# Soft mixture-of-experts stage on one Trainium2 core: token tiles stored tile by tile, transposed through a ring of four quarter-buffers, and two expert-weight loads issued at other places

## Chip, cores, metric

One core of a Trainium2 chip. The metric is the device time in microseconds (us) of one execution of the whole program. Below, TensorE (PE) does matmuls and transposes, VectorE is DVE, ScalarE is ACT, GpSimd is POOL, and SP is the engine whose only work here is to issue DMAs.

## What is computed

Three stages in a row, all in float32: attention over 32 heads with pooled queries, a soft mixture of experts (MoE), and a gated feed-forward layer. The change lies where the second begins.

```python
def _attn_ref(q, k, v):                  # B,H,S,D = 4,8,1152,64; queries pooled by 2 -> 576 rows a head
    q_pool = q.reshape(B, H, S // 2, 2, D).mean(axis=3)
    attn = softmax(q_pool @ k.T / sqrt(D))
    return attn @ v
...
def _moe_ref(x, phi, w1, w2):            # x 2304x512 tokens, 8 experts of 4 slots, w1 8x512x1024, w2 8x1024x512
    logits = x @ phi
    d = np.exp(logits - logits.max(0)); d /= d.sum(0)
    slot_input = d.T @ x                 # 32 slots
    h = np.maximum(slot_input[e] @ w1[e], 0.0); slot_out[e] = h @ w2[e]      # for each expert e
    c = np.exp(logits - logits.max(1)); c /= c.sum(1)
    return c @ slot_out
...
def _moe2_ref(x, w_gate, w_val, w_out, rms_g):                                # d_ff = 1536
    xn = x / rms(x) * rms_g
    return (silu(xn @ w_gate) * (xn @ w_val)) @ w_out
```

## The kernel before

**Attention** runs over 16 pairs of heads (`attention`, an unrolled start, a loop, an unrolled end). Its result stays in SBUF as `x_nat`: 2304 tokens are five tiles (`NI` = 5: four of 128 tokens and a tail of 64) of each of the four batches, 512 channels each. Before the change a pair's five tiles lie side by side in `x_nat`, so one tile's channels are spread over the whole buffer.

**The MoE stage** (`rest`, `slots_tensor`, `slots_scalar`, `slots_vector`, `slots_sync`) first needs logits, so PE transposes each token tile (L1050, `token_transposes`) into one of six PSUM banks, ACT and DVE in turn copy the banks to the SBUF buffers `xt` (L1129, L1130), and PE multiplies them by `phi` (L1063, `logits`), four batches at a time in four column strips of the array. Before the change a job is one batch of one tile with its four channel blocks `c`, and the logits of a whole tile (16 matmuls) follow the 16 transposes of the tile after it. When the last logits are there (`lt_step`), DVE takes the maxima, ACT the exponentials, PE sums the tokens by their weights, tile by tile (L1096, `z_ps`), and `slots_done` says that the 32 slot inputs are ready. Then come the experts, four at a time (`g` = 0, 1): first layer (L1442), transposes, second layer (L1481); and then shares of `w_gate` and `w_val` (L1497), and the main loop of the feed-forward stage (L1624).

**Weights.** All expert weights, 33.5 MB, come from HBM by DMAs issued in program order from SP's one queue. Those of the first four experts go to seven slots and `w2_last` while attention ends. Those of the other four have to wait for a free place; their first layers are loaded by channel block `c`, four experts together, 2 MB each: `w1_first` (c = 0) in attention's block, then `w1_third` (c = 2, in pieces), `w1_second` (c = 1, on top of `x_nat`), then `slots_of_four` (c = 3 and the second layers), `weights`, and the feed-forward weights `w_gv` and `wo_raw`. Each has its wait in SP's program, below.

**Between the two stages** stands a block end (L1908) at which all five engines wait for each other: an engine arrives when its instructions of the block are issued or done, SP when it has issued its last DMA.

```python
        sp.wait_ge(group_ready, s_groups.upto(NPAIR - 1, 1))
        sp.dma_start(mem.w1_first[:], mem.w1_v[4:8, :, 0, :].rearrange("e p f -> p e f")).then_inc(mem.w1_first_in, 16)
    ...
    def slots_sync(sp):
        sp.wait_ge(lt_step, NI)
        sp.dma_start(w1_next[2][:, 0:3, :], ...)
        sp.wait_ge(z_ready, 1)
        sp.dma_start(w1_next[1], ...)
        sp.wait_ge(slots_done, 1)
        sp.dma_start(w1_next[2][:, 3, :], ...)
```

Of the kernel before, what the change touches and what calls it, by code (L numbers as in the profile page):

```python
# [6 lines left out]
P = 128  # L7
# [160 lines left out]
def attention(nc, mem, q, k, v):  # L168
# [221 lines left out]
    def _(sp):  # L390
# [74 lines left out]
        sp.dma_start(mem.w1_first[:], mem.w1_v[4:8, :, 0, :].rearrange("e p f -> p e f")).then_inc(mem.w1_first_in, 16)  # L465

# [314 lines left out]
    def _(dve):  # L781
# [77 lines left out]
        def normalise(at, k):  # L859
# [4 lines left out]
            if at.step is None:  # L864
                where = bass.ds((at.pair - 1) * NI * P, NI * P)
            else:
                where = bass.ds(at.step * (2 * NI * P) + (at.pair - 1) * NI * P, NI * P)
            x_pair = x_nat[:, where].rearrange("p (i h d) -> p i h d", i=NI, h=2)
# [50 lines left out]
def rest(nc, mem, w_gate, w_val, w_out, out):  # L919
# [15 lines left out]
    w1_third = mem.sb("w1_third", [P, 4, F1], FP32)  # L935
    assert mem.at == end_r3
    mem.at = third
# [3 lines left out]
    w1_in = [mem.w1_first_in] + [sem(f"w1_in{c}") for c in range(1, KT)]  # L941
# [36 lines left out]
    mem.at = mem.x_end - 4 * NPAIR * NI * P  # L978
    hid = mem.sb("hid", [P, F1], FP32)
# [3 lines left out]
    w1_second = mem.sb("w1_second", [P, 4, F1], FP32)  # L983
    mem.at -= SLOT
    comb_cat = mem.sb("comb_cat", [P, NI * B, 4, NS], F32R)
    plain_t = mem.sb("plain_t", [P, NTOK + P - TAIL], F32R)
# [15 lines left out]
    x_tiles = x_nat[:, :].rearrange("p (b c i d) -> p b i c d", b=B, c=HP, i=NI)  # L1002
# [22 lines left out]
    xt_jobs = [[(b, i)] for i in range(NF) for b in range(B)] + [[(0, NF), (1, NF)], [(2, NF), (3, NF)]]  # L1025
# [4 lines left out]
    def jobs_of(i):  # L1030
        return range(B * i, B * i + B) if i < NF else range(B * NF, B * NF + 2)
# [9 lines left out]
    def slots_tensor(pe):  # L1041
        def token_transposes(i):
            for n in jobs_of(i):
                if n >= NTB:
                    pe.wait_ge(xt_out_v if n % 2 else xt_out_a, (n - NTB) // 2 + 1)
                rows = rows_of(i)
                for m, (b, _) in enumerate(xt_jobs[n]):
                    for c in range(KT):
                        at = rows * (KT * m + c)
                        last = nc.tensor.transpose(banks[:, n % NTB, at:at + rows], x_tiles[0:rows, b, i, c, :],  # L1050
                                                   ident[0:rows, 0:rows])
                last.then_inc(xt_ready, 1)

        def logits(i):
            if i == 0:
                pe.wait_ge(small_in, 32)
            done = (jobs_of(i)[-1] + 1) // 2
            pe.wait_ge(xt_out_a, done)
            pe.wait_ge(xt_out_v, done)
            rows = rows_of(i)  # L1060
            for c in range(KT):
                for b in range(B):
                    last = nc.tensor.matmul(lt_ps[32 * b:32 * b + 32, P * i:P * i + rows], phi_sb[:, c, :],  # L1063
                                            xt[i % 2][:, c, b, 0:rows],
                                            start=(c == 0), stop=(c == KT - 1), tile_position=(0, 32 * b))
            last.then_inc(lt_step, 1)

        token_transposes(0)
        for i in range(1, NI):
            token_transposes(i)  # L1070
            logits(i - 1)
# [49 lines left out]
    def xt_job_out(engine, copy, n):  # L1121
# [3 lines left out]
        if i >= 2:  # L1125
            engine.wait_ge(lt_step, i - 1)
# [838 lines left out]
```

## Time and profile before

| | |
|---|---|
| three runs, us | 803.42, 804.03, 807.40 (median 804.03) |
| the profiled execution | 807.56 us, of which its span is 805.6 us (1.96 us lie around it) |
| PE, DVE, ACT busy | 786.8, 500.0, 460.9 us |
| granted clock of PE, mean | 0.991 of full |

The span is the time from the first instruction of the program to the last. Attention fills it up to about 540 us, the MoE stage and the preparation of the feed-forward weights go to about 625 us, the feed-forward loop to the end. PE is busy nearly throughout, but "busy" counts a matmul from its start to its modelled end.

### The profile page before, as it was taken

How to read it: one execution, taken by the hardware profiler on the slowest of the kernel's cores; microseconds unless marked ns; L12 is line 12 of the kernel's file. 1: busy time of each engine (PE TensorE's matmuls, PEld its weight loads, DVE VectorE, ACT ScalarE, POOL GpSimd, SP SyncE). 2: the span in 40 equal slices, each digit the busy share in tenths (PEclk: the TensorE clock that was granted, in tenths of full speed). 3: DMA queues.
4: the chain of work that ended last, by engine and by line, in shares of the span. 5: the costliest groups of instructions: out<-in, count | busy, mean ns of one | idle time of the engine just before them, and what ended most of it. 6: DMA issues, size and time to landing. Idle time of an engine off the chain costs nothing. (4 is left out here: it accounts for less than half of the span.)

```text
span 805.6 us, 16312 instructions
## 1 busy us (share of the span) xinstructions
PE 786.8 (98%) x5286; PEld 585.6 (73%) x5286; DVE 500.0 (62%) x967; ACT 460.9 (57%) x873; POOL 181.3 (23%) x243
## 2 busy tenths in 40 slices
PE   7999999999999999999999999989998999999997
PEld 7777777777777777777777777766344888888876
DVE  6766667666666676666756666644325566666665
ACT  5676676676766667666767676642123454434333
POOL 6351331522414325133152240000002330000000
PEclk9999999999999999999999999999998899999999
DMA  8539747365383463744836518586997001010010
GB/s 229 124 88 289 202 104 180 81 150 119 90 201 82 123 157 78 175 103 102 188 74 148 122 34 239 219 290 227 401 400 303 0 1 53 1 52 21 33 52 27
DMA packets 83032, 112.02 MB, mean 139 GB/s; under 512 B 45361, under 2 KB 47409, under 8 KB 82481
## 3 DMA queue, kind: packets, MB, share of 16 engines
q1 hardware_dynamic: 82832, 111.24, 48.7%
q8 instruction: 24, 0.39, 0.2%
q10 hardware_dynamic: 160, 0.26, 0.1%
q14 instruction: 16, 0.12, 0.0%
HBM read 71.37 MB, written 4.72 MB: 94 GB/s over the span
## 5 line engine op out<-in xcount | busy, mean ns | idle before, releaser
L579 PE MATMUL scores<-k_stack,q_stack 128*128 128x384 f32 x960 | 275.1, 376 | 2.8 <-DVE q_stack L796 2.4
L766 ACT COPY pt<-tbank 128x384 f32<-128x384 f32 x288 | 138.2, 480 | 152.8 <-PE tbank L516 152.7
L516 PE MATMUL tbank<-ident,probs 128*128 128x128 f32 x1296 | 219.5, 278 | 0.4 <-ACT probs L738 0.3
L516 PEld LDWEIGHTS tbank<-ident,probs 128*128 128x128 f32 x1296 | 156.5, 140 | 67.8 <-issue 41.9
L738 ACT ACTIVATE probs<-scores,neg_max 128x1152 f32<-128x1152 f32 x144 | 175.9, 1222 | 7.4 <-DVE neg_max L836 3.0
L612 PE MATMUL obank<-pt,v_in 128*64 128x320 f32 (+1 forms) x1152 | 167.3, 417 | 0.9 <-ACT o_t L753 0.9
L832 DVE TENSOR_REDUCE row_max<-scores 128x1 f32<-128x384 f32 x144 | 80.1, 556 | 117.0 <-PE scores L579 115.5
L579 PEld LDWEIGHTS scores<-k_stack,q_stack 128*128 128x128 f32 x960 | 147.8, 191 | 3.8 <-ACT k_stack L378 2.6
L825 DVE TENSOR_REDUCE row_max<-scores 128x1 f32<-128x768 f32 x144 | 136.6, 948 | 2.2 <-PE scores L579 1.6
L612 PEld LDWEIGHTS obank<-pt,v_in 128*64 128x64 f32 x1152 | 72.0, 136 | 58.1 <-issue 25.8
L887 DVE COPY pt<-tbank 128x384 f32<-128x384 f32 x144 | 80.2, 557 | 36.8 <-PE tbank L516 34.1
L343 POOL TENSOR_TENSOR k_hi<-k_lo,one 128x512 fp32r<-128x512 f32 (+1 forms) x45 | 37.2, 826 | 279.6 <-ACT k_lo L683 262.2
L1721 ACT CAST h_hi<-hid 128x512 fp32r<-128x512 f32 (+1 forms) x60 | 34.7, 578 | 102.2 <-DVE hid L1858 102.2
L1624 PE MATMUL banks<-wo_hi,h_hi 128*128 128x512 f32 x216 | 86.2, 399 | 0.6 <-DVE h_lo L1864 0.4
L1624 PE MATMUL banks<-wo_lo,h_hi 128*128 128x512 f32 x216 | 85.1, 394 | 0.0
L1624 PE MATMUL banks<-wo_hi,h_lo 128*128 128x512 f32 x216 | 84.9, 393 | 0.0
L1864 DVE TENSOR_TENSOR h_lo<-hid,h_hi 128x512 fp32r<-128x512 f32 (+1 forms) x60 | 38.3, 639 | 37.9 <-ACT h_hi L1721 37.9
L1809 DVE TENSOR_TENSOR scaled<-banks,inv_rms 128x512 f32<-128x512 f32 (+1 forms) x60 | 38.2, 636 | 27.8 <-PE banks L1536 27.1
L1624 PEld LDWEIGHTS banks<-wo_hi,h_hi 128*128 128x128 f32 x216 | 41.1, 190 | 11.4 <-DVE h_lo L1864 3.3
L1624 PEld LDWEIGHTS banks<-wo_hi,h_lo 128*128 128x128 f32 x216 | 41.1, 190 | 8.8
L1624 PEld LDWEIGHTS banks<-wo_lo,h_hi 128*128 128x128 f32 x216 | 41.2, 191 | 8.1
L348 POOL TENSOR_TENSOR k_lo<-k_lo,k_hi 128x512 fp32r<-128x512 f32 (+1 forms) x45 | 45.4, 1008 | 3.5
(217 smaller groups left out, 702.7 us busy)
## 6 DMA issues: line engine op xcount, KB each, us to landing
weights<-in_moe_w SPq DMA_DIRECT2D x7, 2048.0 KB, 11.4
v_in<-in_v SPq DMA_DIRECT2D x16, 576.0 KB, 4.0
k_in<-in_k SPq DMA_DIRECT2D x30, 288.0 KB, 4.9
k_stack<-k_hi SPq DMA_DIRECT2D x30, 288.0 KB, 3.6
k_stack<-k_lo SPq DMA_DIRECT2D x30, 288.0 KB, 3.6
q_in<-in_q SPq DMA_DIRECT2D x14, 512.0 KB, 5.1
slots_of_four<-in_moe_w SPq DMA_DIRECT2D x12, 512.0 KB, 11.2
q_stack<-q_hi SPq DMA_DIRECT2D x30, 144.0 KB, 3.3
```

The costliest lines, as they stand in the source:

```text
L348: last = ops.tensor_tensor(low[:, cols], low[:, cols].bitcast(FP32), high[:, cols].bitcast(FP32), ALU.subtract)
L516: last = nc.tensor.transpose(tbank[:, bank, cols], src, ident[0:rows, 0:rows])
L579: last = nc.tensor.matmul(scores[:, bank, 0:CH], q_stack[at.par][:, h, order, cols], k_stack[at.par][:, h, keys], start=(x == 0), stop=(x ...
L612: last = nc.tensor.matmul(obank[rows, 0:GROUP_WIDTH[group]], v_in[:, par, h, D * kt:D * kt + D], pt[group][:, h, kt, :], start=(kt == 0), ...
L738: nc.scalar.activation(probs[:, odd, :].rearrange("p (c k) -> p c k", c=3), scores[:, first:first + 3, 0:CH], ACT.Exp, bias=neg_max[:, odd ...
L766: nc.scalar.copy(pt_out(at, e), pt_from(at, e)).then_inc(out_by_act, 1)
L825: nc.vector.tensor_reduce(row_max[:, odd, 0:1], scores[:, first:first + 2, 0:CH], axis=AX.XY, op=ALU.max).then_inc(partial_max, 1)
L832: nc.vector.tensor_reduce(row_max[:, odd, 1:2], scores[:, 2, 0:CH], axis=AX.X, op=ALU.max).then_inc(partial_max, 1)
L887: nc.vector.tensor_copy(pt_out(at, e), pt_from(at, e)).then_inc(out_by_dve, 1)
L1624: last = nc.tensor.matmul(y_ps[:, t, :], a[:, f % 3, cols], w[:, f, :], start=(f == 0 and x == 0), stop=(f == NFT - 1 and x == 2))
L1809: nc.vector.tensor_tensor(scaled[:, f % 2, 0:width], gv_ps[:, f % 2, 0, 0:width], inv_rms[:, columns(n)], ALU.mult).then_inc(scaled_done, 1)
L1864: nc.vector.tensor_tensor(h_lo[:, f % 3, 0:width], hid2[:, f % 2, 0:width], h_hi[:, f % 3, 0:width].bitcast(FP32), ALU.subtract).then_inc( ...
```

## The change

`x_nat` is stored tile by tile: `[P, NI, NPAIR * P]`, so that the first two tiles are one contiguous stretch, exactly as large as `w1_second`, and `w1_second` is put there. A new semaphore `z_step` is raised when the token sums of tiles 0 and 1 are done, and the load of `w1_second` waits for it and no longer for `z_ready`.

The transposed tokens go through a ring of four buffers, each with one channel block of four batches (2 KB a partition, half the room in all). A job is now one (tile, channel block), four transposes and four logit matmuls, and PE's order is four jobs of transposes, then one job's logits and one job's transposes in turn. There are 20 jobs; `lt_step` counts all of them. This frees the place of two of the four experts of `w1_third` during attention: their load, 1 MB, is issued in attention's block, right behind `w1_first`; the third expert's is issued after the last logits, alone.

```diff
         sp.dma_start(mem.w1_first[:], mem.w1_v[4:8, :, 0, :].rearrange("e p f -> p e f")).then_inc(mem.w1_first_in, 16)
+        sp.dma_start(mem.w1_third[:, 0:2, :], mem.w1_v[4:6, :, 2, :].rearrange("e p f -> p e f")).then_inc(mem.w1_third_in, 16)
...
-            x_pair = x_nat[:, where].rearrange("p (i h d) -> p i h d", i=NI, h=2)
+            x_pair = x_nat[:, :, where].rearrange("p i (h d) -> p i h d", h=2)
...
-    xt = [mem.sb(f"xt{n}", [P, KT, B, P], FP32) for n in range(2)]
+    xt = mem.sb("xt", [P, 4, B, P], FP32)
...
-    xt_jobs = [[(b, i)] for i in range(NF) for b in range(B)] + [[(0, NF), (1, NF)], [(2, NF), (3, NF)]]
+    xt_jobs = [(i, c) for i in range(NI) for c in range(KT)]
...
     def slots_sync(sp):
-        sp.wait_ge(lt_step, NI)
-        sp.dma_start(w1_next[2][:, 0:3, :], mem.w1_v[4:7, :, 2, :].rearrange("e p f -> p e f")).then_inc(w1_in[2], 16)
-        sp.wait_ge(z_ready, 1)
+        sp.wait_ge(lt_step, len(xt_jobs))
+        sp.dma_start(w1_next[2][:, 2, :], mem.w1_v[6, :, 2, :]).then_inc(w1_in[2], 16)
+        sp.wait_ge(z_step, 1)
         sp.dma_start(w1_next[1], mem.w1_v[4:8, :, 1, :].rearrange("e p f -> p e f")).then_inc(w1_in[1], 16)
         sp.wait_ge(slots_done, 1)
         sp.dma_start(w1_next[2][:, 3, :], mem.w1_v[7, :, 2, :]).then_inc(w1_in[2], 16)
...
+        def token_transposes(n):
+            i, c = xt_jobs[n]
+            rows = rows_of(i)
+            if n >= NTB:
+                pe.wait_ge(xt_out_v if n % 2 else xt_out_a, (n - NTB) // 2 + 1)
+            for b in range(B):
+                last = nc.tensor.transpose(banks[:, n % NTB, rows * b:rows * b + rows], x_tiles[0:rows, b, i, c, :],
+                                           ident[0:rows, 0:rows])
+            last.then_inc(xt_ready, 1)
...
+            pe.wait_ge(xt_out_v if n % 2 else xt_out_a, n // 2 + 1)
+            for b in range(B):
+                last = nc.tensor.matmul(lt_ps[32 * b:32 * b + 32, P * i:P * i + rows], phi_sb[:, c, :],
+                                        xt[:, n % 4, b, 0:rows],
+                                        start=(c == 0), stop=(c == KT - 1), tile_position=(0, 32 * b))
...
+        for n in range(len(xt_jobs)):
+            token_transposes(n)
+            if n >= 3:
+                logits(n - 3)
+        for n in range(len(xt_jobs) - 3, len(xt_jobs)):
+            logits(n)
...
+            if i == 1:
+                last.then_inc(z_step, 1)
```

How instructions move on PE, where the MoE stage begins. A row is a run of equal instructions; transposes read `x_nat` and `ident`, logit matmuls read `xt` and `phi_sb`. Before:

```order
L1050 MATMUL banks<-ident,x_nat 128x128 x32
L1063 MATMUL banks<-xt_4097,phi_sb 32x128 x16
L1050 MATMUL banks<-ident,x_nat 128x128 x16
L1063 MATMUL banks<-xt_4098,phi_sb 32x128 x16
L1050 MATMUL banks<-ident,x_nat 128x128 x16
L1063 MATMUL banks<-xt_4097,phi_sb 32x128 x16
```

And after the change, the first rows of the same place:

```order
L1047 MATMUL banks<-ident,x_nat 128x128 x16
L1058 MATMUL banks<-xt,phi_sb 32x128 x4
L1047 MATMUL banks<-ident,x_nat 128x128 x4
L1058 MATMUL banks<-xt,phi_sb 32x128 x4
L1047 MATMUL banks<-ident,x_nat 128x128 x4
L1058 MATMUL banks<-xt,phi_sb 32x128 x4
```

The same 80 transposes and 80 logit matmuls stand there; before they alternate in runs of 16, after it in runs of 4 up to the last transposes.

On SP, at the end of attention's block and the start of the next one, before:

```order
125 L465 DMA w_first<-in_moe_w 128x4x1024 [waits group_ready]
126 L1908 UNCONDITIONAL_BRANCH
127 L1366 UNCONDITIONAL_BRANCH [waits barrier_Pool_Activation_PE_DVE_SP_release]
128 L1035 DMA w_third<-in_moe_w 128x3x1024 [waits lt_step]
129 L1037 DMA w_second<-in_moe_w 128x4x1024 [waits z_ready]
130 L1039 DMA w_third<-in_moe_w 128x1024 [waits slots_done]
```

And after the change (the names are cut to their stem: `w_third` is `w1_third`):

```order
125 L465 DMA w_first<-in_moe_w 128x4x1024 [waits group_ready]
126 L466 DMA w_third<-in_moe_w 128x2x1024
127 L1901 UNCONDITIONAL_BRANCH
128 L1359 UNCONDITIONAL_BRANCH [waits barrier_Pool_Activation_PE_DVE_SP_release]
129 L1034 DMA w_third<-in_moe_w 128x1024 [waits lt_step]
130 L1036 DMA w_second<-in_moe_w 128x4x1024 [waits z_step]
131 L1038 DMA w_third<-in_moe_w 128x1024 [waits slots_done]
```

One more DMA is issued before the block end, for which all five engines wait, and the one behind the block end is a third as large.

## Rows read from the trace of the kernel before

**Rows 1.** Chain that ended last, in order of time: start us, us, what

```profile
593.75 19.74 DMA w_gv<-in_moe_w_val
613.53 0.85 PE banks L1497 x8
...
625.56 4.88 PE banks L1624 x12
...
630.89 2.74 PE banks L1624 x12
```

**Rows 2.** SP's DMA issues, 496 to 540 us: start us, us, line, DMA

```profile
496.93 10.22 SPq L454 DMA_DIRECT2D phi_sb<-in_moe_phi  x1
...
537.21 1.89 SPq L465 DMA_DIRECT2D w_first<-in_moe_w  x1
```

**Rows 3.** Timeline of all engines round the block end, 537 to 540 us

```profile
537.79 0.74 PE L516 MATMUL tbank<-ident,o_t 128*128 128x128 f32 x5 [0.61 <-ACT o_t L753]
...
539.24 0.29 DVE L875 TENSOR_TENSOR x_nat<-tbank,tail_inv 64x128 f32<-64x128 f32 x1
...
539.86 0.96 PE L1050 MATMUL banks<-ident,x_nat 128*128 128x128 f32 x7 [1.34 <-PEq L1908]
```

**Rows 4.** Timeline of transposes, logit matmuls and copies, 539 to 548 us

```profile
539.83 3.48 PEld L1050 LDWEIGHTS banks<-ident,x_nat 128*128 128x128 f32 x32 [1.55 <-issue]
...
543.48 0.81 PEld L1063 LDWEIGHTS banks<-xt,phi_sb 128*32 128x32 f32 x32 [0.17 <-issue]
...
543.59 0.69 DVE L1129 COPY xt<-banks 128x512 f32<-128x512 f32 x1 [0.18 <-PE banks L1050]
544.49 1.73 PEld L1050 LDWEIGHTS banks<-ident,x_nat 128*128 128x128 f32 x16 [0.20 <-issue]
...
547.40 0.64 PEld L1050 LDWEIGHTS banks<-ident,x_nat 128*128 128x128 f32 x6 [0.20 <-issue]
```

**Rows 5.** SP's DMA issues behind the block end, 550 to 600 us

```profile
553.11 0.37 SPq L1035 DMA_DIRECT2D w_third<-in_moe_w  x1
561.48 0.37 SPq L1037 DMA_DIRECT2D w_second<-in_moe_w  x1
...
565.42 0.37 SPq L1373 DMA_DIRECT2D slots_of_four<-in_moe_w  x1
567.14 15.72 SPq L1383 DMA_DIRECT2D slots_of_four<-in_moe_w  x12
...
591.87 2.50 SPq L1393 DMA_DIRECT2D w_gv<-in_moe_w_val  x4
```

**Rows 6.** Timeline of PE, token sums of tiles 1 to 4

```profile
557.64 3.77 PE L1096 MATMUL banks<-x_nat,exp_l 128*32 128x512 f32 x32
```

**Rows 7.** Stretches: busy us by engine (x count), granted clock, DMA share, GB/s

```profile
559.00:562.00 3.00, 2.90 (x27) 0.71 (x20) 0.65 (x1) 0.51 (x2) 0.00 (x0) 1.00 0.00 0
565.00:570.00 5.00, 5.00 (x52) 1.43 (x44) 3.45 (x21) 1.02 (x2) 0.00 (x0) 1.00 1.03 413
```

**Rows 8.** Timeline of PE, 598 to 614 us

```profile
598.47 1.92 PE L1481 MATMUL banks<-weights,hid_t 128*32 128x512 f32 x16 [0.46 <-DMA weights<-in_moe_w]
...
603.91 1.47 PE L1497 MATMUL banks<-w_gv,st_scaled 128*32 128x384 f32 x16
...
609.75 0.85 PE L1497 MATMUL banks<-w_gv,st_scaled 128*32 128x384 f32 x8 [0.74 <-DMA w_gv<-in_moe_w_val]
...
611.63 0.85 PE L1497 MATMUL banks<-w_gv,st_scaled 128*32 128x384 f32 x8
```

**Rows 9.** Stretches as in Rows 7, at 5, at 9 and at 620 us

```profile
5.40:8.80 3.40, 1.05 (x10) 0.84 (x9) 1.49 (x7) 1.91 (x4) 0.50 (x2) 1.00 1.13 233
8.80:12.20 3.40, 3.40 (x14) 3.30 (x15) 2.20 (x4) 0.44 (x1) 3.24 (x7) 0.50 0.88 275
619.70:623.10 3.40, 3.40 (x10) 2.19 (x8) 2.99 (x5) 0.95 (x2) 0.00 (x0) 0.51 0.09 36
```

**Rows 10.** Timeline of PE at the program's start

```profile
8.70 2.18 PE L579 MATMUL scores<-k_stack,q_stack 128*128 128x384 f32 x6 [2.35 <-DVE q_stack L796]
```

More of the change, by code:

```diff
@@ L934, in rest @@
     mem.at = third = r3 + 2 * SLOT
-    w1_third = mem.sb("w1_third", [P, 4, F1], FP32)
-    assert mem.at == end_r3
-    mem.at = third
-    xt = [mem.sb(f"xt{n}", [P, KT, B, P], FP32) for n in range(2)]
+    w1_third = mem.w1_third
+    mem.at = third + 2 * 4 * F1
+    xt = mem.sb("xt", [P, 4, B, P], FP32)
     assert mem.at == end_r3
     w2_last_in = mem.w2_last_in
-    w1_in = [mem.w1_first_in] + [sem(f"w1_in{c}") for c in range(1, KT)]
+    w1_in = [mem.w1_first_in, sem("w1_in1"), mem.w1_third_in, sem("w1_in3")]
     w2_in = [sem(f"w2_in{n}") for n in range(4)]
@@ L978, in rest @@
     mem.at = mem.x_end - 4 * NPAIR * NI * P
+    w1_second = mem.sb("w1_second", [P, 4, F1], FP32)
+    assert mem.at == mem.x_end - 4 * (NI - 2) * NPAIR * P
+    mem.at -= SLOT
+    comb_cat = mem.sb("comb_cat", [P, NI * B, 4, NS], F32R)
+    plain_t = mem.sb("plain_t", [P, NTOK + P - TAIL], F32R)
     hid = mem.sb("hid", [P, F1], FP32)
@@ L1041, in slots_tensor @@
     def slots_tensor(pe):
[L1042 to L1052, printed above, removed]
@@ L1054, in logits @@
-        def logits(i):
-            if i == 0:
-                pe.wait_ge(small_in, 32)
[L1057 to L1065, printed above, removed]
-            last.then_inc(lt_step, 1)
@@ L1068, in slots_tensor @@
[L1068 to L1071, printed above, removed]
-        logits(NF)
+        def token_transposes(n):
[7 more added lines that the diff above has]
+            last.then_inc(xt_ready, 1)
@@ new lines, in logits @@
+        def logits(n):
+            i, c = xt_jobs[n]
+            rows = rows_of(i)
+            if n == 0:
+                pe.wait_ge(small_in, 32)
+            pe.wait_ge(xt_out_v if n % 2 else xt_out_a, n // 2 + 1)
[3 more added lines that the diff above has]
+                                        start=(c == 0), stop=(c == KT - 1), tile_position=(0, 32 * b))
+            last.then_inc(lt_step, 1)
@@ L1074, in keep_busy @@
+        for n in range(len(xt_jobs)):
[4 more added lines that the diff above has]
+            logits(n)
         def keep_busy():
-            nc.tensor.matmul(banks[:, NTB - 1, :], ident[:], x_nat[:, 0:NF * P], start=True, stop=True)
+            nc.tensor.matmul(banks[:, NTB - 1, :], ident[:], x_nat[:, 0, 0:NF * P], start=True, stop=True)
         keep_busy()
@@ L1121, in xt_job_out @@
     def xt_job_out(engine, copy, n):
-        i = xt_jobs[n][0][1]
-        rows = rows_of(i)
+        rows = rows_of(xt_jobs[n][0])
         engine.wait_ge(xt_ready, n + 1)
-        if i >= 2:
-            engine.wait_ge(lt_step, i - 1)
-        first, count = xt_jobs[n][0][0], len(xt_jobs[n])
-        if count == 1:
-            return copy(xt[i % 2][:, :, first, :], banks[:, n % NTB, :].rearrange("p (c t) -> p c t", c=KT))
-        return copy(xt[i % 2][:, :, first:first + count, 0:rows],
-                    banks[:, n % NTB, 0:rows * KT * count].rearrange("p (b c t) -> p c b t", b=count, c=KT))
+        if n >= 4:
+            engine.wait_ge(lt_step, n - 3)
+        return copy(xt[:, n % 4, :, 0:rows], banks[:, n % NTB, 0:rows * B].rearrange("p (b t) -> p b t", b=B))
     def slots_scalar(act):
@@ L1437, in _ @@
                 if g:
-                    pe.wait_ge(w1_in[c], 32 if c == 2 else 16)
+                    pe.wait_ge(w1_in[c], 48 if c == 2 else 16)
                 for n in range(2):
@@ L1923, in build @@
         mem.w1_first = mem.sb("w1_first", [P, 4, F1], FP32)
+        mem.w1_third = mem.sb("w1_third", [P, 4, F1], FP32)
+        mem.w1_third_in = mem.sem("w1_in2")
         mem.w2_last_in, mem.w1_first_in, mem.small_in = mem.sem("w2_last_in"), mem.sem("w1_in0"), mem.sem("small_in")
```

17 lines of the change are left out of this document (6 added, 11 removed).

## Prediction

> **What bounds the kernel now.** I read the chain that ended last first. In the stretch that the change touches it runs over the DMA queue: from about 567 us SP's issues stand in it, then one wait for a load, 19.74 us up to 613.49, behind which PE starts the last share of `w_val` at 613.53 [rows 1]. From 565 us on the DMA engines move 413 GB/s at a share of 1.03, so they are full, while between 559 and 562 us they move nothing [rows 7]. So here the end is set by the time at which the queue becomes full for good. That is the load of `w1_second`, issued at 561.48, with `w1_first` long issued and 1.5 MB of `w1_third` issued at 553.11 [rows 5]. All later loads follow without a gap.
>
> PE stands close behind. Between 598 and 614 us it waits for loads before 598.47 (0.46 us), before 609.75 (0.74) and before the last share (613.53, while the one before it ended at 611.63 + 0.85 = 612.48: 1.05) [rows 1, 8]. Each wait also lays open the tail of the matmuls in front of it, which otherwise lies under the next ones: one share takes 0.85 us, two in a row 1.47 and not 1.70 [rows 8], so 0.2 us each. Without waits PE would be 0.46 + 0.74 + 1.05 + 3 x 0.2 = 2.9 us earlier at the last share. An earlier DMA stream is worth something up to there, and a PE that comes more than 2.9 us late costs something.
>
> **Gain: the two loads.** `w1_second` no longer waits for all token sums but for those of tiles 0 and 1. The sums of tiles 1 to 4 take 3.77 us from 557.64 on [rows 6]; a quarter of that and the 0.2 us of a matmul's tail end at 558.7, and the old signal comes at 561.41. The issue is **2.7 us earlier relative to PE**. The 1 MB of `w1_third` issued in attention fills idle time of the queue before that point, and what has to go through after it is the same as before; so it adds nothing to the 2.7 (the queue is empty when `w1_second` is issued, before and after). Later issues wait for PE at `w1_used`, the first at 565.42 [rows 5], 4 us behind the old issue and 6.7 behind the new one; `w1_second` and a quarter of `w1_third` (2.6 MB, 6.4 us at 413 GB/s) just cover that. If nothing else moved, the end would come 2.7 us earlier.
>
> **Cost 1: the block end.** The new DMA stands between `w1_first` and the block end, for which all five engines wait. SP's `w1_first` is issued at 537.21 and takes 1.89 us, to 539.10, where a free queue takes 0.37 [rows 2, 5]. The last other engine is DVE, ready at 539.53, and PE starts 0.33 us later, at 539.86 [rows 3]. So SP has 0.4 us to spare. What does one more issue take? The rows show that an issue returns when the DMA in front of it has been passed on to the DMA engines: `phi_sb`, only 64 KB, took 10.22 us behind three loads of 2 MB [rows 2]. They also show that the room is counted in pieces, not bytes: four loads of 0.79 MB in 128 pieces of 6 KB took 0.63 us each, while the engines were still moving pieces of 2 KB (128 of these are 0.26 MB, 0.64 us at 413 GB/s; 0.79 MB would be 1.9 us) [rows 5]. In front of the new DMA stands `w1_first` with 512 pieces of 4 KB, the queue is full at 539.10 (that issue had to wait), and what it is moving are the 2 KB pieces of `w2_last`: 512 of these are 1.05 MB, 2.6 us. So SP is ready at about 541.75 and PE starts near 542.1, **2.2 us later**. Bounds: 0.37 us if there is room after all (no delay beyond 0.1), 1.3 us if only the new DMA's own 256 pieces count (delay 0.9), 5.1 us if bytes count (2.1 MB; delay 4.7). I take 2.2, since the pieces fit two kinds of rows.
>
> The Trainium skill ("DMA: Bandwidth & Descriptors", Issuing engines are not separate DMA queues) says that the sequencer's time to initiate a DMA is usually small relative to the DMA itself. By that the block end would not move, and the sum below would be 2.2 us less; the 1.89 us of the issue in front speaks against it here.
>
> **Cost 2: changes between transposes and logit matmuls.** Both kinds are unchanged in number and size. PE's weight loads show what a change between them costs. 32 transposes' loads take 3.48 us, 0.109 each; but from the transposes at 544.49 to those at 547.40 pass 2.91 us, with 16 transposes (1.74) and 16 logit matmuls (eight steps of four loads, 0.87 at 0.109 a step) in them. 0.3 us are left for one change there and back; the rows show them as 0.17 us without a load before the logit matmuls and 0.20 before the transposes [rows 4]. Before there are 3 such round trips and a last change there; after there are 16 and a last one. **13 x 0.3 = 3.9 us.** Copies don't bind: 0.69 us for a DVE copy [rows 4], one for every two jobs, and two jobs now take 2 x (0.44 + 0.22 + 0.3) = 1.9 us of PE. The ring is no limit either, since a buffer's reader is issued before the transposes that feed its next writer. At the end the last logits wait for the copy behind the last transposes: about 0.2 us more than now. Bounds: nothing, if PE hides the changes when they come every half microsecond, and 4.8 us (13 x 0.37) if the two gaps count in full.
>
> **Cost 3: PE's clock.** Today PE stands idle for 1.34 us at the block end [rows 3]; after the change from 538.53 to 542.1, 3.5 us. At the program's start 2.35 us of idleness [rows 10] in a stretch with 1.05 us of PE work were followed by 3.4 us at a granted clock of 0.50 (1.2 GHz) [rows 9]. In those 3.4 us the transposes would run at half speed: **1.7 us**. Bounds: nothing, and 5 us for ten us at 0.50, as it is in this trace from 620 us on. This is the least certain term.
>
> The Trainium skill ("TensorE: Matmul & The Clock Gate", Why this matters for your kernels) warns of idle gaps of over about 3 us between bursts of matmuls; the trace agrees, with a fall after 2.35 us already.
>
> **The sum.** PE's chain from the block end on is 2.2 + 3.9 + 0.2 + 1.7 = 8.0 us late at the token sums. Loads follow it less 2.7, PE itself less 2.9, so the end moves by the larger, 8.0 - 2.7 = **+5.3 us**. Everything behind, `wo_raw` too, comes with the same queue and shifts alike.
>
> Against which time? The profiled execution took 807.56 (805.6 of span and 1.96 around it), 3.5 us above the median of 804.03. It holds some ten us at 0.50 after 619.7 [rows 9], in which the first step of the feed-forward loop took 4.88 us and later ones 2.74 [rows 1]: 2.1 us there, and about as much again in the matmuls before it. I take it that the two runs at 803.4 and 804.0 lack that stretch, and that the changed kernel's median lacks it as well. By its own span the sum gives 812.9, by the median 804.03 + 5.3 = **809.3**, which I predict.
>
> **Rivals.**
> - *No clock fall at the block end*, costs 1 and 2 as worked out: 6.3 - 2.7 = +3.6, 807.6. For it: PE's 1.34 us of idleness today leaves the clock at 1.00.
> - *Only one of the costs comes.* Changes hidden, block end late: 4.1 - 2.7 with the clock term, less than nothing without it: 803.7 to 805.4. Block end on time, changes paid: 4.1 - 2.7, 805.4. For the first: a logit matmul's loads are short (0.81 us for 32) [rows 4] and PE has four jobs to choose from.
> - *The change does what it says* (the other side): SP's issue returns within its 0.4 us and the changes are hidden; the stream is full 2.7 us earlier, PE can follow by 2.9: 0.2 - 2.7, 801.5. It decides from the point where costs 1 to 3 together stay under 2.7 us. That is 0.3%, so even this one is hardly to be told from no change.
> - *Worse*: an issue that counts bytes (+2.5), or a clock that stays at 0.50 for ten us: 812 to 815.
>
> **Chances.** Forecast 0.42, no clock fall 0.22, only one cost 0.20, the change as meant 0.08, worse 0.08. The range has to reach into the third case and the lower edge of the last: 803.3 to 811.8. A measurement of this kernel tells about 0.5%, 4.0 us, from no change: slower means over 808.05. Of the forecast nearly all lies there, of the no-fall case a fifth, and the worse case: 0.50. Faster (under 800.0) needs more than the 2.7 us that the loads can give: 0.05. The same: 0.45.
>
> **What would show it.** Of cost 1: the issue of the new `w1_third` DMA takes about 2.6 us, and PE's idleness before its first transposes is 3.5 us, not 1.3. Of cost 2: from one run of four transposes to the next about 0.95 us, and from the first transposes to the end of the logits 17 us (13.2 now) at full clock. Of cost 3: a granted clock of 0.50 for some us behind 542. Of the gain: 2.7 us less between the last logits' end and the issue of `w1_second` than the 8.4 now, and PE waiting for loads in 598 to 620 about as often as today. I am wrong if that issue takes under 0.5 us, or if the span of transposes and logits stays near 13 us.

## The result: 1.0% slower

The changed kernel takes 812.32 us (median of four, 811.66 to 816.08), the one before 803.72 on the same chip (median of four, 803.00 to 807.40): ratio 1.0101, 95% interval 1.0066 to 1.0136. I had forecast slower, but 809.3 with an upper end of 811.8. The profiled execution took 811.71, of which 809.8 are its span. Here and below the ratio with its interval is worked out from all executions of both kernels; it is not the quotient of the two medians and can differ from it by 0.0018.

**The block end.** SP's DMA issues in the changed kernel (start us, us, line, DMA):

```profile
536.42 1.89 SPq L465 DMA_DIRECT2D w_first<-in_moe_w  x1
538.35 2.58 SPq L466 DMA_DIRECT2D w_third<-in_moe_w  x1
561.18 0.34 SPq L1034 DMA_DIRECT2D w_third<-in_moe_w  x1
566.84 0.37 SPq L1036 DMA_DIRECT2D w_second<-in_moe_w  x1
571.48 0.34 SPq L1038 DMA_DIRECT2D w_third<-in_moe_w  x1
573.49 0.37 SPq L1366 DMA_DIRECT2D slots_of_four<-in_moe_w  x1
575.21 14.57 SPq L1376 DMA_DIRECT2D slots_of_four<-in_moe_w  x12
```

The new issue takes 2.58 us (538.35). Between 538.4 and 540.9 the DMA engines moved 511 packets, all but a few of 2 KB, so `w_first`, with its 512 pieces of 4 KB, was waiting behind a load of 2 KB pieces, as the prediction had it. Round the block end, the timeline of VectorE and TensorE:

```profile
538.46 0.29 DVE L876 TENSOR_TENSOR x_nat<-tbank,tail_inv 64x128 f32<-64x128 f32 x1
...
541.38 1.94 PE L1047 MATMUL banks<-ident,x_nat 128*128 128x128 f32 x8 [3.65 <-PEq L1901]
```

VectorE is done at 538.46 + 0.29 = 538.75. PE starts 2.63 us behind it, where it was 0.33 [rows 3]: the block end comes 2.3 us later. PE has waited 3.65 us and not 1.34.

**Transposes and logits.** The timeline of PE's weight loads in the middle of them:

```profile
549.11 0.42 PEld L1047 LDWEIGHTS banks<-ident,x_nat 128*128 128x128 f32 x4 [0.20 <-issue]
...
549.69 0.16 PEld L1058 LDWEIGHTS banks<-xt,phi_sb 128*32 128x32 f32 x8 [0.17 <-issue]
...
550.05 0.42 PEld L1047 LDWEIGHTS banks<-ident,x_nat 128*128 128x128 f32 x4 [0.20 <-issue]
```

One run of four transposes follows the one before by 0.94 us (549.11 to 550.05), and the two gaps of 0.17 and 0.20 us without a load stand in each cycle. The whole stretch, 541.38 to 561.12, takes 19.74 us; before, 13.19. Part of the longer stretch is the clock. Stretches of the changed kernel (busy us with counts of PE, PE's weight loads, DVE, ACT, POOL; then granted clock, busy share of the DMA engines, GB/s):

```profile
540.50:547.30 6.80, 5.92 (x37) 4.52 (x38) 2.32 (x9) 1.76 (x3) 0.00 (x0) 0.50 1.05 401
547.30:561.10 13.80, 13.76 (x205) 8.61 (x205) 5.00 (x8) 3.68 (x7) 0.00 (x0) 1.00 0.36 143
629.20:632.60 3.40, 3.13 (x7) 2.48 (x8) 1.72 (x3) 1.82 (x5) 1.28 (x1) 0.50 0.00 0
```

The clock was at 0.50 (1.2 GHz) for 6.8 us behind the wait, and once more for 3.4 us at 629. In the profile of before it stood at 0.50 for 10.2 us from 619.7 on, which [rows 9] shows a part of.

**The weight stream.** `w_second` is issued 5.7 us after the last logits' end (561.12 to 566.84), before 8.4 (553.05 to 561.48): the 2.7 us are there. The chain that ended last still runs through the last load of `w_val`, as in [rows 1]:

```profile
600.76 19.84 DMA w_gv<-in_moe_w_val
620.64 0.85 PE banks L1490 x8
...
631.12 3.52 PE banks L1617 x12
635.10 2.72 PE banks L1617 x12
```

It lands at 620.60, before at 613.49, and PE waits for it as before (1.11 us, before 1.05). The first step of the feed-forward loop takes 3.52 us here and 4.88 in [rows 1], since the clock comes back at 632.6. But counted from the last logits' end that is 59.48 against 60.43 us: of 2.7 us only 0.95 have arrived. Where the others went is seen in the stretches. Four stretches from 5.5, 8.5, 12 and 15 us behind the last logits on, up to 19, first the kernel before, then the changed one:

```profile
558.55:561.55 3.00, 3.00 (x30) 0.73 (x23) 0.94 (x2) 0.06 (x1) 0.00 (x0) 1.00 0.00 0
561.55:565.05 3.50, 3.26 (x29) 1.72 (x31) 1.93 (x4) 0.58 (x2) 0.00 (x0) 1.00 0.73 248
565.05:568.05 3.00, 3.00 (x32) 0.91 (x28) 2.86 (x20) 0.74 (x1) 0.00 (x0) 1.00 1.02 416
568.05:572.05 4.00, 3.78 (x36) 1.47 (x32) 1.35 (x3) 1.19 (x2) 0.00 (x0) 1.00 1.03 408
```

```profile
566.62:569.62 3.00, 3.00 (x30) 0.72 (x23) 0.95 (x2) 0.06 (x1) 0.00 (x0) 1.00 0.51 188
569.62:573.12 3.50, 3.26 (x29) 1.72 (x31) 1.92 (x4) 0.59 (x2) 0.00 (x0) 1.00 1.02 417
573.12:576.12 3.00, 3.00 (x32) 0.91 (x28) 2.86 (x20) 0.74 (x1) 0.00 (x0) 1.00 0.86 288
576.12:580.12 4.00, 3.78 (x36) 1.47 (x32) 1.35 (x3) 1.19 (x2) 0.00 (x0) 1.00 0.98 348
```

PE, VectorE and ScalarE do the same in each pair of rows. The DMA engines start earlier in the changed kernel (188 GB/s instead of 0, 417 instead of 248), but then fall to 288 and 348 GB/s, where they moved 416 and 408 before. At 12 us the queue holds little: `w_second` has landed at +12.9, half a megabyte of `w_third` at +14.4. The loads behind are issued at +12.4, +14.1 and +14.5 (573.49, 575.21 and on), when PE's expert layers release their places, and these moments are the same before: 565.42 and 567.14 in [rows 5] are +12.4 and +14.1. The low rate lasts to +19, longer than the queue is short: the 2 MB of `slots_of_four` stand in it from +12.7 on.

When the 16 engines finish shows where the rest is lost. Each reports its part of the last `w_val` load by itself, and the load has landed with the last report. Times of the reports behind the last logits:

| kernel | first engine | mean of 16 | last engine (landed) |
|---|---|---|---|
| before | 58.1 | 58.81 | 60.4 |
| changed | 56.3 | 57.46 | 59.5 |
| `e11_after_again` | 56.5 | 57.51 | 59.4 |
| `e3_both` | 56.8 | 58.10 | 60.7 |
| `e7_z_ready` | 58.5 | 58.95 | 60.4 |
| `e8_third_after` | 57.4 | 58.09 | 59.3 |
| `e9_z_only` | 56.5 | 57.86 | 60.7 |
| `e10_backlog` | 59.3 | 59.84 | 61.4 |

In the changed kernel the mean engine is 1.35 us earlier than before, so half of the 2.7 us has got through the dip; but the engines are further apart, 3.2 us from first to last and not 2.3, and the last one is only 0.95 earlier.

Each execution, before and after, counted from the end of VectorE's last attention instruction:

| kernel | to first transpose | transposes and logits (at 0.50) | last logits to `w_val` landed | sum | clock at 0.50 behind 619 |
|---|---|---|---|---|---|
| before | 0.33 | 13.19 (0) | 60.43 | 73.95 | 10.2 |
| changed | 2.63 | 19.74 (6.8) | 59.48 | 81.85 | 3.4 |
| `e11_after_again` | 1.77 | 18.67 (3.4) | 59.44 | 79.88 | 6.8 |
| `e1_third_behind` | 0.33 | 17.06 (0) | 60.18 | 77.57 | 3.4 |
| `e2_runs_of_16` | 2.44 | 15.40 (3.4) | 60.60 | 78.44 | 6.8 |
| `e3_both` | 0.39 | 15.45 (3.4) | 60.69 | 76.53 | 6.8 |
| `e4_swap` | 1.19 | 18.51 (3.4) | 58.48 | 78.19 | 10.2 |
| `e5_warm` | 1.97 | 17.06 (0) | 59.86 | 78.89 | 3.4 |
| `e6_late_third` | 0.33 | 13.79 (0) | 60.96 | 75.08 | 6.8 |
| `e7_z_ready` | 0.33 | 15.45 (3.4) | 60.38 | 76.16 | 10.2 |
| `e8_third_after` | 0.33 | 13.79 (0) | 59.32 | 73.44 | 0 |
| `e9_z_only` | 0.33 | 13.19 (0) | 60.65 | 74.17 | 0 |
| `e10_backlog` | 0.42 | 14.85 (3.4) | 61.40 | 76.67 | 3.4 |

All in us, one profiled execution each. The experiments in it come below. A warning on the column of the landing: seven of these kernels (changed, `e11`, `e1` to `e5`) have the same program behind the last logits, and it still ranges from 58.48 to 60.69 (the mean engine from 57.25 to 58.39). A difference of 1 us in the landing between two single executions is thus no finding by itself.

### The profile page after: what moved, and what is told of

Same layout as the page of the kernel before. It is cut to its first block and busy times, and to the rows that moved or that the text cites. A ratio compares the mean times of both kernels' runs of the same rounds, so it can differ in the third digit from the quotient of the medians.

```text
span 809.8 us, 16317 instructions
## 1 busy us (share of the span) xinstructions
PE 791.0 (98%) x5286; PEld 585.7 (72%) x5286; DVE 498.7 (62%) x968; ACT 461.3 (57%) x874; POOL 181.6 (22%) x243
## 5 line engine op out<-in xcount | busy, mean ns | idle before, releaser
L613 PEld LDWEIGHTS obank<-pt,v_in 128*64 128x64 f32 x1152 | 72.0, 136 | 58.1 <-issue 25.8
```

The lines of the kernel that those rows point to most:

```text
L613: last = nc.tensor.matmul(obank[rows, 0:GROUP_WIDTH[group]], v_in[:, par, h, D * kt:D * kt + D], pt[group][:, h, kt, :], start=(kt == 0), ...
```

## Experiments

All edits are to the changed kernel unless said otherwise; ratios are to the kernel before on the same chip.

### The two costs taken out: the load behind the block end, longer runs

`e1_third_behind` takes the new load out of attention's block and issues it as the first thing behind the block end, in `slots_sync`.

```diff
-        sp.dma_start(mem.w1_third[:, 0:2, :], ...)
...
+        sp.dma_start(mem.w1_third[:, 0:2, :], ...)
         sp.wait_ge(lt_step, len(xt_jobs))
```

> The changed kernel with one line moved: the 1 MB load of w1_third is issued as the first DMA behind the block end and no longer in front of it. Theory (the issue holds up the block end, and the long idleness lets PE's clock fall): the first transposes start 0.33 us behind DVE's last instruction again, PE is idle 1.3 us there and not 3.65, the clock stays at 1.00 behind it, and the logits take 17 us and not 19.8. The time falls by 2.3 + 2.9 = 5.2 us, from 812.3 to about 807, which is 2 to 3.5 us above the kernel before (the changes between transposes and logit matmuls stay). Rival (the issue is harmless, all the loss is in the finer jobs): 812.

`e2_runs_of_16` keeps that load and orders PE's work in runs of four jobs.

```diff
-        for n in range(len(xt_jobs)):
-            token_transposes(n)
-            if n >= 3:
-                logits(n - 3)
-        for n in range(len(xt_jobs) - 3, len(xt_jobs)):
-            logits(n)
+        for n in range(6):
+            token_transposes(n)
+        for first in range(0, len(xt_jobs), 4):
+            for n in range(first, first + 4):
+                logits(n)
+            for n in range(first + 6, min(first + 10, len(xt_jobs))):
+                token_transposes(n)
```

> The changed kernel with the same jobs, buffers and loads, but PE's program in runs of four jobs: transposes of jobs 0 to 5, then logits 0 to 3, transposes 6 to 9, logits 4 to 7, and so on: 4 round trips between the two kinds and not 16. Theory (a change there and back costs 0.3 us at full clock): 12 x 0.3 = 3.6 us less, 812.3 to about 808.7; the issue of the new DMA still takes 2.6 us and the clock still falls. Rival (the finer jobs cost through their waits on copies, or through nothing): the logits take as long as in the changed kernel, 19.8 us, and the time stays at 812.

`e3_both` has both edits.

> Both at once: the 1 MB load behind the block end, and runs of four jobs. Theory: costs 1 to 3 of the prediction are gone but for 0.5 us, and what is left is the gain of the two loads: if all of the 2.7 us counts, 803.7 - 2.2 = 801.5; if the DMA stream runs dry again before the next load may be issued, as it does in the changed kernel's trace (1.7 us lost), 803.2. Rival (something else in the change, such as the new layout of x_nat, costs as well): above 804.5.

Measured: `e1_third_behind` 809.54 us, 1.0054 (1.0032 to 1.0077); `e2_runs_of_16` 809.46, 1.0043 (1.0022 to 1.0064); `e3_both` 805.74, 1.0004 (0.9982 to 1.0026); before 806.66 on the same chip. The times expected were counted from 803.7 for the kernel before, which is 3 us less than it took here, so the ratios have to be compared. Expected were about 1.004 and 1.006, and both intervals hold these. For `e3_both` its interval shuts out the 0.997 of a full gain, and holds both the 0.999 of a gain partly lost and the rival's 1.001. Each edit takes about half of the loss, together they take all of it. The table shows by which stage: the first one puts the first transpose back to 0.33 us, and with it the clock stayed at 1.00 and the stretch took 17.06; the second shortens the stretch to 15.40 with 3.4 us at 0.50 in it. So cost 1 (with the clock that falls behind it) and cost 2 are shown as causes. Even `e3_both` isn't measurably faster than before, though it issues `w_second` 2.7 us earlier.

### The clock

`e5_warm` puts twelve small matmuls of `ident` at the end of PE's program for attention; they fill the wait at the block end (538.19 to 541.03 in the trace).

```diff
         each_pair(pe, pair, ends=(NPAIR,))
+        for n in range(12):
+            nc.tensor.matmul(obank[:, 0:P], ident[:], ident[:], start=True, stop=True)
```

> The changed kernel with 12 matmuls of ident by ident more at the end of PE's part of attention (2.6 us of work whose result nobody reads), so that PE is idle about 1 us and not 3.65 at the block end; the new DMA still holds it up by 2.3 us. Theory (the idleness makes the clock fall, and the fall costs the transposes about 2.9 us): granted clock 1.00 behind the block end, logits in 17 us, time 812.3 - 2.9 = 809.4. Rival (the clock falls for another reason, or its fall is hidden by the loads): 812.

Measured: 811.42 us, 1.0075 (1.0047 to 1.0102). PE waits 0.30 us instead of 3.65, the clock stays at 1.00, the stretch takes 17.06 us, as in `e1_third_behind`. So in the two executions of the changed kernel the fall cost 19.74 - 17.06 = 2.7 us (6.8 us at 0.50) and 18.67 - 17.06 = 1.6 (3.4 us). The time tells less. Its ratio is the expected one (809.4 to 803.7 is 1.007), but the interval also holds the rival's 1.010 and overlaps those of the unaltered changed kernel (1.0066 to 1.0136 and 1.0058 to 1.0117). The price of the fall rests on the traces.

`e11_after_again` is the changed kernel without any edit.

> The changed kernel once more, unaltered, to see what of its stages repeats. Expected: issue of w_third 2.6 us, first transpose 2.6 us after VectorE's last attention instruction, four transposes and four logit matmuls in 0.94 us at the full clock, w_second 5.7 us after the last logits, w_val[3] at 58.5 to 60.7 us after them. Open: how long the clock stays at 0.50 after the wait at the block end, 3.4 us or 6.8. The time: 1.0% above before.

Measured: 812.55 us, 1.0088 (1.0058 to 1.0117). All stages repeat but two: the clock's 3.4 us instead of 6.8, and a block end 1.4 us late and not 2.3, because attention itself ended later against SP's queue here.

But a wait need not be long. `e7_z_ready` and `e8_third_after` (below) run the same program up to the last logits. Timeline of PE's first transposes and one stretch, first `e7_z_ready`:

```profile
539.22 4.04 PE L1047 MATMUL banks<-ident,x_nat 128*128 128x128 f32 x20 [1.34 <-PEq L1902]
```

```profile
539.50:542.90 3.40, 3.40 (x19) 3.40 (x18) 1.53 (x7) 1.17 (x2) 0.00 (x0) 0.50 1.05 399
```

and `e8_third_after`:

```profile
539.92 2.81 PE L1047 MATMUL banks<-ident,x_nat 128*128 128x128 f32 x24 [1.34 <-PEq L1902]
```

```profile
539.60:543.00 3.40, 3.08 (x36) 2.95 (x40) 2.32 (x9) 1.17 (x2) 0.00 (x0) 1.00 1.05 403
```

The same wait of 1.34 us, as in [rows 3]; behind it the clock fell to 0.50 in one execution and not in the other, and 24 transposes take 2.81 us or 20 of them 4.04. The Trainium skill ("TensorE: Matmul & The Clock Gate", Why this matters for your kernels) advises against idle gaps of over about 3 us; here the clock fell behind gaps of 1.34, 1.41 and 1.43 us (`e7_z_ready`, `e3_both`, `e10_backlog`), and it stayed behind the same 1.34 us in five other executions (before, `e1_third_behind`, `e6_late_third`, `e8_third_after`, `e9_z_only`). What PE did just before doesn't tell them apart: in the 4.5 us before the first transpose it was busy for 2.55 us in `e7_z_ready` and for 2.55 or 2.56 in those five. Behind longer gaps it fell each time: 2.21 us (`e4_swap`), 2.79, 3.45 (`e2_runs_of_16`) and 3.65. The fall after 2.35 us at the program's start, which the prediction took for agreement with the skill, also lies under 3 us.

### Which pieces an issue waits for

`e4_swap` issues the new load in front of `w1_first`.

```diff
-        sp.dma_start(mem.w1_first[:], ...)
         sp.dma_start(mem.w1_third[:, 0:2, :], ...)
+        sp.dma_start(mem.w1_first[:], ...)
```

> The changed kernel with its two last DMA issues of attention's block in the other order: the 1 MB load of w_third (256 pieces) first, w_first (512 pieces) second. Theory A (an issue waits until the DMA in front of it has been passed on, so the wait goes by the pieces of that one): the second issue takes about 1.3 us instead of 2.6, the first about 1.9 as now, PE's first transpose follows VectorE's last attention instruction by about 1.3 us instead of 2.6, and the kernel is about 1.3 us faster than the changed one: about 811.0. Theory B (the wait goes by the room that the issued DMA itself needs, 512 pieces now): the second issue takes 2.6 us or more, and the time stays at 812.3 or grows.

Measured: 809.27 us, 1.0055 (1.0037 to 1.0073). SP's two issues:

```profile
536.44 1.80 SPq L465 DMA_DIRECT2D w_third<-in_moe_w  x1
538.28 1.23 SPq L466 DMA_DIRECT2D w_first<-in_moe_w  x1
```

The DMA that is issued second now has 512 pieces of its own and 256 in front of it, and takes 1.23 us instead of 2.58. So the wait goes by the pieces of the DMA in front, as worked out from [rows 2, 5]. The first transpose comes 1.19 us behind VectorE (2.63 in the changed kernel). The ratio is 0.0033 to 0.0046 under that of the changed kernel (1.0088, 1.0101), 2.7 to 3.7 us, where 1.3 us was expected: in the trace the clock was at 0.50 for 3.4 us only behind the block end, and the stream was the shortest of all, which the edit doesn't explain: behind the last logits the program is unchanged.

### Where the 2.7 us went

`e7_z_ready` is `e3_both` with the wait for all token sums again.

```diff
-        sp.wait_ge(z_step, 1)
+        sp.wait_ge(z_ready, 1)
```

> The kernel with the w_third load behind the block end and transposes and logits in runs of four jobs (805.7 us before this), with one thing undone: the load of w_second waits for all token sums again, so it is issued about 8.4 us after the last logits instead of 5.7. Theory A (the weight queue runs empty before the loads that wait for the expert layers, whose issue times at +12.4, +14.1, +14.5 us don't move, so the earlier load only makes an emptier queue): w_val[3] lands 60.5 to 61.0 us after the last logits, as with the early load (60.7), and the time is the same within 0.5 us. Theory B (the early load gives its 2.7 us, and something else takes them, the place of w_second or of the ring): w_val[3] lands 2.7 us later, at 63.4, and the time is about 808.4.

Measured: 807.52 us, 1.0021 (0.9997 to 1.0045). `w_second` is issued at +8.4, and `w_val` lands 60.38 us after the last logits, in `e3_both` 60.69: theory A on the landing, where B said 63.4. The mean engine is 0.85 us later than in `e3_both`, and the times of the two (1.0021 and 1.0004) can't be told apart; B's 2.7 us would be 1.0038, which the interval doesn't shut out either. Here the trace decides, not the time. The place of `w_second` and the ring are here as in the changed kernel, and neither makes the stream longer.

`e9_z_only` is the kernel before with this part alone: `x_nat` by tiles, `w_second` on its first two, issued at `z_step`.

```diff
-        sp.wait_ge(z_ready, 1)
+        sp.wait_ge(z_step, 1)
         sp.dma_start(w1_next[1], ...)
```

> The kernel before with one part of the change alone: x_nat stored tile by tile, w_second on its first two tiles, and its load issued when the token sums of tiles 0 and 1 are done. The jobs, the xt buffers and the loads of w_third are those of before. Theory A (the queue runs empty anyway before the loads that wait for the expert layers): w_second is issued 5.7 us after the last logits instead of 8.4, w_val[3] lands at 59.5 to 60.7 after them (60.4 before), and the time is that of before within 0.7 us. Theory B (the early load gives its 2.7 us in full): w_val[3] lands at 57.7, and the time is about 801.

Measured: 805.35 us, 1.0005 (0.9984 to 1.0026), which shuts out the 0.997 of theory B. SP's issues, the four stretches, and the chain's wait for `w_val`:

```profile
552.82 0.37 SPq L1038 DMA_DIRECT2D w_third<-in_moe_w  x1
558.49 0.37 SPq L1040 DMA_DIRECT2D w_second<-in_moe_w  x1
563.12 0.34 SPq L1042 DMA_DIRECT2D w_third<-in_moe_w  x1
565.14 0.37 SPq L1378 DMA_DIRECT2D slots_of_four<-in_moe_w  x1
```

```profile
558.27:561.27 3.00, 3.00 (x30) 0.72 (x23) 0.94 (x2) 0.07 (x1) 0.00 (x0) 1.00 0.59 198
561.27:564.77 3.50, 3.27 (x29) 1.72 (x31) 1.93 (x4) 0.58 (x2) 0.00 (x0) 1.00 1.02 411
564.77:567.77 3.00, 3.00 (x32) 0.91 (x28) 2.86 (x20) 0.74 (x1) 0.00 (x0) 1.00 0.80 303
567.77:571.77 4.00, 3.78 (x36) 1.47 (x32) 1.36 (x3) 1.20 (x2) 0.00 (x0) 1.00 0.91 300
```

```profile
593.51 19.92 DMA w_gv<-in_moe_w_val
```

Issued 2.7 us earlier, landed at 613.43, which is 60.65 us after the last logits; before 60.43. The DMA engines are ahead of those of before up to +12 and lose it again up to +19: 303 and 300 GB/s against 416 and 408, which is (113 x 3 + 108 x 4) KB = 0.77 MB, 1.9 us at 410 GB/s. Up to +28 (395 GB/s before and 393 here from +19 on) the sums over the stretches are 7.30 and 7.68 MB, so 0.9 us of the lead are left. They are still there at the end, but not in the landing: the mean engine reports its part of the last `w_val` load 0.95 us earlier than before (57.86 against 58.81), the last one 0.2 us later, since the engines are spread over 4.2 us and not 2.3. `e7_z_ready` and `e10_backlog`, the other kernels without a dip, have spreads of 1.9 and 2.1 us. So the dip takes some 1.8 of the 2.7 us and the engines that fell out of step take what is left.

`e8_third_after` is `e3_both` with the third expert's half megabyte behind `w_second` instead of in front of it.

```diff
-        sp.dma_start(w1_next[2][:, 2, :], ...)
         sp.wait_ge(z_step, 1)
         sp.dma_start(w1_next[1], ...)
+        sp.dma_start(w1_next[2][:, 2, :], ...)
```

> The kernel with the w_third load behind the block end and transposes and logits in runs of four jobs, with the half-megabyte load of the third expert of w_third issued behind w_second (5.7 us after the last logits) instead of in front of it (0.1 us after). Theory A (the queue runs empty between +12 and +16 us, so half a megabyte more there costs nothing): w_val[3] lands 60.7 us after the last logits, within 0.3, and the dip in the DMA rate at +13 to +15 us is filled. Theory B (the bytes and the queue's rate decide, and the low rate there has another cause): it lands 1.3 us later, at 62.0, and the dip stays.

Measured: 805.17 us, 1.0012 (0.9990 to 1.0034). `w_val` lands at 59.32, not later but 1.4 us earlier than in `e3_both`, with half a megabyte more to move; the rate from +12 to +15 is 374 GB/s (264 in `e3_both`). The mean engine is where it was (58.09 against 58.10), so 0.5 MB, 1.3 us of queue, cost nothing: theory A. The 1.4 us are the last engine's alone.

`e10_backlog` is `e9_z_only` with all 1.5 MB of `w_third` behind `w_second`.

```diff
-        sp.dma_start(w1_next[2][:, 0:3, :], ...)
         sp.wait_ge(z_step, 1)
         sp.dma_start(w1_next[1], ...)
+        sp.dma_start(w1_next[2][:, 0:3, :], ...)
```

> The kernel before with x_nat stored by tiles and w_second on its first two tiles, issued after the token sums of tiles 0 and 1 (5.7 us after the last logits), and with the 1.5 MB load of w_third behind it instead of in front of it. The queue then has 1.5 MB more to move from that moment on. Theory A (the loads behind, which PE's expert layers release at +12.4, +14.1 and +14.5 us, find an almost empty queue when w_second is early, and that is what takes the gain): with this backlog there is no dip at +12 to +15 us and no slow packets up to +19, the rate stays at 400 KB/us and more, and w_val[3] lands at 60.4 to 61.5 although 1.5 MB (3.9 us) more follow w_second: about the time of before, up to 1 us more. Rival B (the rate falls at +12 us whatever the queue holds, because of what PE and the other engines do then): the dip stays, and w_val[3] lands at about 64.

Measured: 807.31 us, 1.0034 (1.0011 to 1.0058). SP's issues and the same four stretches:

```profile
559.49 0.37 SPq L1039 DMA_DIRECT2D w_second<-in_moe_w  x1
559.90 0.50 SPq L1040 DMA_DIRECT2D w_third<-in_moe_w  x1
564.07 0.34 SPq L1042 DMA_DIRECT2D w_third<-in_moe_w  x1
566.08 0.37 SPq L1378 DMA_DIRECT2D slots_of_four<-in_moe_w  x1
```

```profile
559.22:562.22 3.00, 3.00 (x30) 0.72 (x23) 0.93 (x2) 0.08 (x1) 0.00 (x0) 1.00 0.56 193
562.22:565.72 3.50, 3.26 (x29) 1.70 (x31) 1.94 (x4) 0.58 (x3) 0.00 (x0) 1.00 1.03 418
565.72:568.72 3.00, 3.00 (x32) 0.91 (x28) 2.86 (x20) 0.73 (x1) 0.00 (x0) 1.00 1.03 415
568.72:572.72 4.00, 3.78 (x36) 1.48 (x32) 1.36 (x3) 1.19 (x2) 0.00 (x0) 1.00 1.01 410
```

PE's work in these stretches is that of every other kernel (32 and 36 matmuls from +12 to +19), and the loads behind are released at the same +12.4. But the queue is full, and the rate is 415 and 410 GB/s. `w_val` lands at 61.40, where theory A said 60.4 to 61.5 and B 64: 1.5 MB more, 3.8 us of queue, cost 0.75 us against `e9_z_only` in the landing and 2.0 in the mean engine. The other 1.8 is what the dip had taken. So what PE and the others do at +12 us is not the cause of the dip; how much the queue holds when they are released is. The slower packets belong to it: from +12 to +19 the engines are busy for 0.80 to 0.91 of the time in `e9_z_only`, but move 303 and 300 GB/s and not 0.80 and 0.91 of 410. Why packets take longer there is open, and so is why this goes on to +19, though 2 MB have stood in the queue again since +12.7.

### What is left of the change

`e6_late_third` has no early load of `w_third` and the runs of four jobs: the ring, the storing by tiles and the early `w_second` are left.

> The changed kernel without its early load (w_third's first three experts in one load after the last logits, as before the change) and with transposes and logits in runs of four jobs, so only the ring, the storing by tiles and the early load of w_second are left of it. Theory A (the three costs are the early load's issue, the changes between transposes and logits, and the clock that falls when PE has waited at the block end; the early loads give nothing): PE's first transpose follows VectorE's last attention instruction by 0.33 us, the time from it to the last logits is 13.8 us without a fall of the clock (13.2 before), w_val[3] lands about 60.5 after them, and the time is that of before plus 0.6 us. Rival B (the early load of w_third is worth something by itself: a megabyte less after the last logits, 2.6 us of queue): w_val[3] lands 2 us or more later after the last logits than in the kernels that have it (59.3 to 60.7), and the time is over 2 us above before.

Measured: 805.28 us, 1.0002 (0.9975 to 1.0029). First transpose at 0.33, stretch 13.79, `w_val` 60.96 after the last logits, in kernels with the early megabyte 58.5 to 60.7. The mean engine reports at 57.84, in `e3_both` at 58.10. The early load of `w_third` gains nothing that these runs can show. No version here is shown to be faster than the kernel before.

## Why the prediction was right and wrong

- **Cost 1, block end: right.** 2.2 us said, 2.3 measured (1.4 in the second execution). The issue took 2.58 us for 2.6 expected, and `e4_swap` shows that it goes by the DMA in front. The sentence of the Trainium skill that was set against it ("DMA: Bandwidth & Descriptors", Issuing engines are not separate DMA queues: the time to initiate a DMA is usually small) doesn't hold for a full queue: 2.58 us, of which 2.3 stood in the way of five engines.
- **Cost 2, changes: right.** 3.9 us said, and 0.2 for the copy at the end; 17.06 - 13.19 = 3.87 for both measured at full clock. Runs of four jobs make 13.79: 3.27 us for 12 round trips, 0.27 each. The Trainium skill ("TensorEngine Tiling (Array Packing)", Key Properties) states that changing the tiling mode drains TensorE; the gaps of 0.17 and 0.20 us between full-width transposes and matmuls in four column strips fit that, though no run here separates a drain from other causes of the gaps.
- **Cost 3, clock: right in kind.** 1.7 us said, 2.7 and 1.6 measured in the two executions. It fell behind all four gaps of 2.21 to 3.65 us, but how long it then stayed at 0.50 differed between two executions of the same kernel.
- **The gain: wrong; this is the step of the prediction that failed.** 2.7 us said, 1.0 measured. "`w1_second` and a quarter of `w1_third` (2.6 MB, 6.4 us at 413 GB/s) just cover that" took the queue to be moving at the full rate until the gated load at +12.4 and to go on at once. In fact the rate falls from +12 on, to 288 GB/s instead of 416, and stays low up to +19 (348 instead of 408). And the sum counted a stream, where the landing is that of the last of 16 engines, which are further apart behind such a dip. Of 2.7 us 1.0 was left in both executions of the changed kernel, and nothing between before and `e9_z_only`, or between `e7_z_ready` and `e3_both`.
- **Sum.** At the last `w_val` +5.3 was said; 81.85 - 73.95 = +7.9 and 79.88 - 73.95 = +5.9 were measured: 2.3 + 3.9 + 2.7 - 1.0 and 1.4 + 3.9 + 1.6 - 1.0.
- **Against which time: the second step that failed.** "I take it that ... the changed kernel's median lacks it as well", the late stretch at 0.50. From the landing to the end of the span it takes 187.7 us without such a stretch (`e9_z_only`), 189.2 with 3.4 us of it, 190.6 with 6.8 and 192.1 with 10.2. Of the changed kernel's 12 runs nine have a mean clock of 0.994 or less, which is some 10 us at 0.50, more than the 6.8 and 3.4 us behind the block end in the two traces. So most of them have another stretch; in the two traces it is 3.4 and 6.8 us late, and 3.4 us at the start of the second.
- **How much of the 8.6 us is clock.** The 80 runs of before beside the experiments, time against mean granted clock, lie along a line from 803.1 us at 1.000 with 5.7 us more for each 0.01 less; the 12 of the changed kernel along one from 808.6 with 5.4. At the same mean clock the change costs 5.3 to 5.5 us (standard error 1.0 at 1.000), which within that error fits costs 1 and 2 less the gain: 1.4 to 2.3, 3.9, less 1.0, together 4.3 to 5.2. Forecast without the clock were 3.6, so the missing 1.7 of the gain is nearly all of the difference. The other 3 us of the 8.6 are a lower clock (0.9925 in the mean of 12 runs, while a run of before at 803.7 belongs to 0.999), of which 1.7 was forecast. The fall behind the block end accounts for 1.6 to 2.7 of them; whether the change also makes the clock fall more often elsewhere isn't settled. The first four runs of before, three of them at 803.0 to 804.0, were a lucky draw: the 80 later ones had medians of 805.3 to 806.7, against which the changed kernel is 0.9% slower.

The rivals: without a fall of the clock at the block end the ratio is 1.0075 (`e5_warm`), 809.7 us for a kernel before at 803.7, and not 807.6: that rival counted the same gain in full and the same clock elsewhere. The measured time lies in "worse", and more time at 0.50 was indeed part of it (10.2 us in the trace, though only 6.8 of them behind the block end); the byte-counting issue was not. That the forecast said "slower" and came within 3 us rests on two costs that were right and one gain that was not.

## What to carry over

An earlier issue is worth only what the queue can still move until the next load that waits for somebody: follow the stream to that load's issue, and ask what stands in the queue then. Look at all the engines of a load, since the last one sets its landing. A DMA issue just ahead of a point where all engines meet costs the time of the DMA in front of it, if the queue is full; put it behind that point or the short one first. A ring of smaller buffers is paid in changes between two kinds of matmul, here 0.27 us each round trip: halve the buffer, not the run.

## What I had not expected of the hardware

- The clock fell behind a wait of only 1.34 us in `e7_z_ready` and 1.43 in `e10_backlog`, and not behind the same 1.34 us in five other executions. The late stretches at 0.50 lasted 3.4, 6.8 or 10.2 us and cost 1.5, 2.9 and 4.4 us.
- DMA engines that are busy 0.91 of the time moved 300 GB/s in `e9_z_only`, where the queue had run thin at +12, and 410 at 1.01 in `e10_backlog`, where it had not, with packets of the same 4 KB.
- The 16 engines reported one 0.79 MB load 1.9 to 2.3 us apart behind a queue that never thinned, and 1.9 to 4.4 us apart behind one that did (`e8_third_after`, `e6_late_third`).
- Behind an empty queue a load of 2 MB landed 7.1 us after its issue (566.84 to 573.98), 2.0 more than its 5.1 us at 413 GB/s. The Trainium skill ("DMA: Bandwidth & Descriptors", Anatomy of one DMA) gives a fixed part of about 2.0 us for a DMA of GpSimd's path; this one, of SP's, agrees.
